# Token numbers copied in FFN units, turn counts loaded once per pair, third row group used from unit 12

## What is computed

```
q_p, k_p = phi(q), phi(k)            # phi: [exp(xW - m), exp(-(xW - m))], m = max|xW|
attn = (q_p @ (k_p.T @ v)) / (q_p . sum(k_p) + 1e-6)
e_idx = argmax(x @ w_gate)           # x = attn; one of 8 experts for each token
out[tokens of e] = gate * sigmoid(x @ w_output_gate)[e] * (relu(x @ w1[e]) @ w2[e])
xn = x / rms(x) * rms_g              # second layer: x = out, d_ff = 1536
y  = (silu(xn @ w_gate) * (xn @ w_val)) @ w_out
```

## Time and profile before

| | us |
|---|---|
| median of 3 runs | 875.22 |
| lowest, highest | 873.22, 879.47 |
| the profiled execution | 873.63 |
| its span | 871.9 |
| attention and routing | 0 to 214 |
| experts' steps | 214 to 445 |
| FFN units | 445 to 730 |
| output tiles | 730 to 872 |

### The profile page before, as it was taken

The page is one execution under the profiler, slowest core; times in us unless marked ns, Lnnn a source line. Parts: engine busy times, 40 slices in busy tenths (PEclk is TensorE's granted clock), DMA queues, the critical chain, the costliest instruction groups (busy, mean ns, idle before and its releaser), DMA issues.

```text
span 871.9 us, 16594 instructions
## 1 busy us (share of the span) xinstructions
PE 840.2 (96%) x6216; PEld 757.3 (87%) x6217; DVE 538.9 (62%) x934; ACT 347.3 (40%) x547; POOL 161.4 (19%) x169
## 2 busy tenths in 40 slices
PE   8999999998988999999989999999999999999997
PEld 6685867767988999999989999999999998888885
DVE  5688786989766954445569777666765774212210
ACT  4544454573155533322354443333433443212211
POOL 1010302112350433203421031111110000101101
PEclk9999999999999999999999999999999999999999
DMA  8613713112349544554662852232421945343320
GB/s 285 209 57 138 275 54 108 55 38 75 127 175 267 227 114 97 141 148 150 184 230 77 280 180 79 79 80 79 142 71 54 357 150 184 123 139 125 125 101 36
DMA packets 65226, 122.41 MB, mean 140 GB/s; under 512 B 9200, under 2 KB 43120, under 8 KB 62480
## 3 DMA queue, kind: packets, MB, share of 16 engines
q1 hardware_dynamic: 57600, 91.98, 34.3%
q0 software_dynamic: 3488, 17.85, 5.3%
q10 hardware_dynamic: 4080, 11.80, 3.9%
HBM read 77.54 MB, written 44.09 MB: 139 GB/s over the span
## 4 chain that ended last, share of the span: by engine, by line
PE 78%; DVE 11%; issue 6%; DMA 2%; ACT 1%; DVEq 1%; SPq 0%; another core or an unknown queue 0%; POOLq 0%; POOL 0%; ACTq 0%
PE ps L1207 9%; PE ps L1209 9%; PE ps L1208 9%; PE ps L1259 5%; PE ps L1258 5%; PE ps L1260 5%; PE ps L956 3%; PE ps L1115 3%; PE ps L1116 3%; PE ps L1117 3%; PE ps L1128 3%; PE ps L1130 3%; PE ps L1129 3%; PE ps L1011 3%; PE ps L916 2%
## 5 line engine op out<-in xcount | busy, mean ns | idle before, releaser
L1207 PE MATMUL ps<-sH,tb 128*128 128x384 f32 x504 | 171.0, 339 | 5.9 <-DVE val L2018 2.9
L1208 PE MATMUL ps<-sL,tb 128*128 128x384 f32 x504 | 170.0, 337 | 0.0
L1209 PE MATMUL ps<-sH,tb 128*128 128x384 f32 x504 | 169.9, 337 | 0.0
L1207 PEld LDWEIGHTS ps<-sH,tb 128*128 128x128 f32 x504 | 95.0, 189 | 8.5 <-DVE val L2018 4.9
L1208 PEld LDWEIGHTS ps<-sL,tb 128*128 128x128 f32 x504 | 95.1, 189 | 0.1
L1209 PEld LDWEIGHTS ps<-sH,tb 128*128 128x128 f32 x504 | 95.2, 189 | 0.0
L2036 DVE TENSOR_TENSOR hTL<-h_st,hTH 128x768 fp32r<-128x768 f32 x36 | 33.0, 954 | 97.4 <-ACT hTH L1516 97.4
L1260 PE MATMUL ps<-woH,hTL 128*128 128x512 f32 x216 | 84.1, 389 | 0.0
L1259 PE MATMUL ps<-woL,hTH 128*128 128x512 f32 x216 | 84.1, 389 | 0.0
L1258 PE MATMUL ps<-woH,hTH 128*128 128x512 f32 x216 | 84.0, 389 | 0.0
L1115 PE MATMUL ps<-xmH,w1H 128*128 128x288 f32 x256 | 76.8, 300 | 5.9 <-issue 2.8
(11 more groups left out here) (246 smaller groups left out, 1784.8 us busy)
## 6 DMA issues: line engine op xcount, KB each, us to landing
h_dram<-hid SPq DMA_DIRECT2D x36, 384.0 KB, 2.8
h_st<-h_dram SPq DMA_DIRECT2D x18, 768.0 KB, 4.1
t_dram<-tb SPq DMA_DIRECT2D x6, 1792.0 KB, 5.7
t_raw<-in_ffn_up SPq DMA_DIRECT2D x13, 512.0 KB, 3.2
tb<-t_dram ACTq DMA_DIRECT2D x6, 1024.0 KB, 6.7
xin<-xs_dram SPq DMA_DIRECT2D x9, 578.2 KB, 9.3
xs_dram<-zrow SPq DMA_DIRECT2D x8, 578.2 KB, 7.9
qT<-in_q SPq DMA_DIRECT2D x4, 1152.0 KB, 5.8
```

The costliest lines, as they stand in the source:

```text
L1207: e.matmul(to, wh, xh, start=(fresh and c == 0), stop=False, skip_group_check=True)
L1208: e.matmul(to, wh, xl, start=False, stop=False, skip_group_check=True)
L1209: done = e.matmul(to, wl, xh, start=False, stop=(c == 1), skip_group_check=True)
```

## The change

1. **Counts.** `turn_of` becomes `turns_of`: both turns' counts are loaded at the begin of a pair (4 loads, on VectorE 5), and none between a pair's turns.
2. **SP's step.** `rows_out(n)` now stands ahead of `step_weights_in(n+2)`, and `numbers_out` is out of the loop.
3. **Numbers.** They are copied at units 6, 8, ... 20, one step each, right behind that unit's `hidden_out`; further steps, if there are any, at unit 21. The numbers are read at unit 23 (before 15) and converted at unit 25 (before 17).
4. **Begin of the FFN.** `group_in(0)` ahead of `operands_in(0)`; `operands_in(1)` waits for the first high part (`s_hi0`) in place of the last hidden chunk.
5. **Around unit 4.** `rows_out(last)`, its waits and `group_in(2)` now stand ahead of `hidden_out(4)`.
6. **Order of units.** (3,0) (3,1) (4,0) (4,1) (5,0) (5,1) (3,2) (4,2) (5,2) in place of (3,0) (3,1) (4,0) (4,1) (3,2) (4,2) (5,0) (5,1) (5,2): group 2 is used from unit 12. Its splits move by two units (from 8A..10B to 10A..12B). `MADE_AT[6]` goes from 13 to 14, and the raw load of visit 6 now follows unit 12 in place of unit 10.
7. **Semaphores.** The sums have one semaphore per group. Group 2's sums stay on GpSimd, with the same waits.

```diff
-MADE_AT = {6: 13, 7: 16, ...
-UNITS = ([(v, sg) for sg in range(2) for v in range(3)] + [(3, 0), (3, 1), (4, 0), (4, 1), (3, 2), (4, 2)]
-         + [(v, sg) for v in range(5, 9) for sg in range(NSG)]
+MADE_AT = {6: 14, 7: 16, ...
+UNITS = ([(v, sg) for sg in range(2) for v in range(3)] + [(v, sg) for v in range(3, 6) for sg in range(2)]
+         + [(v, 2) for v in range(3, 6)] + [(v, sg) for v in range(6, 9) for sg in range(NSG)]
...
+NUMBERS_AT = tuple(range(6, 6 + 2 * (NTOK // G), 2))
...
-        def turn_of(e, x):
-            tiles = e.value_load(tab[0:1, bass.ds(x + TILES, 1)], ...)
-            first = e.value_load(tab[0:1, bass.ds(x + FIRST, 1)], ...)
-            return tiles, first
+        def turns_of(e, pair):
+            return [(e.value_load(tab[0:1, bass.ds(pair * 2 + (par + TILES), 1)], ...),
+                     e.value_load(tab[0:1, bass.ds(pair * 2 + (par + FIRST), 1)], ...))
+                    for par in range(2)]
...
             with e.Fori(0, pairs) as pair:
-                for par in range(2):
-                    tiles, first = turn_of(e, pair * 2 + par)
+                counts = turns_of(e, pair)
+                for par, (tiles, first) in enumerate(counts):
                     with e.If(tiles > 0):
...
                 rows_next(n + 2)
                 weights_out(n + 1)
+                rows_out(n, column_of(n))
                 step_weights_in(n + 2)
-                rows_out(n, col)
-                numbers_out(n, col, row)
...
-            e.wait_ge(s["e_st"], 16 * 8)
-            operands_in(0)
             e.wait_ge(s["xst"], total * 16)
             group_in(0)
-            rows_out(prior, prior_col)
-            e.wait_ge(s["pe_s1"], total * FC)
+            e.wait_ge(s["e_st"], 16 * 8)
+            operands_in(0)
+            rows_out(prior, column_of(prior))
+            e.wait_ge(s["s_hi0"], 1)
             operands_in(1)
...
             for u in range(NU):
-                hidden_out(u)
                 if u == ROOT_AT + 1:
                     rows_out(last, last_col)
                     e.wait_ge(s["s_lo"], 7)
                     e.wait_ge(s["xst"], total * 16 + 32)
                     group_in(2)
+                hidden_out(u)
...
+                if u in NUMBERS_AT:
+                    n = NUMBERS_AT.index(u)
+                    if n > 0:
+                        e.wait_ge(s["idst"], n * 16)
+                    e.dma_start(ids_dram[bass.ds(column_of(n), G), :], xs_dram[bass.ds(row_of(n), G), DM:DM + 1])...
```

More of the change, by code:

```diff
@@ L307, in build_program @@
             "FFN up weights of a step: loaded, sums, operands split, stored": "e_in e_add e_hi e_lo e_st",
-            "FFN rows loaded (one per group), their sums, operands split": "x_in0 x_in1 x_in2 s_add s_add1 s_hi0 s_hi s_lo",
+            "FFN rows loaded (one per group), their sums, operands split": "x_in0 x_in1 x_in2 s_add0 s_add1 s_add2 s_hi0 s_hi s_lo",
             "FFN up operands loaded (two parts per buffer)": "t_a0 t_a1 t_a2 t_b0 t_b1 t_b2",
@@ L413, in piece_of @@
             return w1[:, n, :] if n < KC else w2[:, 2 * (n - KC):2 * (n - KC) + 2, :].rearrange("p c n -> p (c n)")
-        def turn_of(e, x):
-            tiles = e.value_load(tab[0:1, bass.ds(x + TILES, 1)], min_val=0, max_val=NTOK // G)
-            first = e.value_load(tab[0:1, bass.ds(x + FIRST, 1)], min_val=0, max_val=NTOK // G + E)
-            return tiles, first
+        def turns_of(e, pair):
+            return [(e.value_load(tab[0:1, bass.ds(pair * 2 + (par + TILES), 1)], min_val=0, max_val=NTOK // G),
+                     e.value_load(tab[0:1, bass.ds(pair * 2 + (par + FIRST), 1)], min_val=0, max_val=NTOK // G + E))
+                    for par in range(2)]
         def is_early(e):
@@ L460, in sums_done @@
         def sums_done(sg, n):
-            return (s["s_add1"], n) if sg == 1 else (s["s_add"], 4 * (sg // 2) + n)
+            return s[f"s_add{sg}"], n
         def nth_load(v):
@@ L579, in rows_next, with numbers_out @@
                 rows_in(row)
-            def numbers_out(n, col, row):
-                e.wait_ge(s["idst"], n * 16 + 16)
+            def numbers_out(n):
+                e.wait_ge(s["idst"], n * 16)
                 settle(e, "carry_sp")
                 with nc.allow_non_contiguous_dma(reason="token numbers"):
-                    e.dma_start(ids_dram[bass.ds(col, G), :], xs_dram[bass.ds(row, G), DM:DM + 1])\
+                    e.dma_start(ids_dram[bass.ds(column_of(n), G), :], xs_dram[bass.ds(row_of(n), G), DM:DM + 1])\
                         .then_inc(s["idst"], 16)
@@ L669, in _ @@
             operands_in(2)
-            last_col, last_row = column_of(last), row_of(last)
+            last_col = column_of(last)
             for u in range(NU):
-                hidden_out(u)
                 if u == ROOT_AT + 1:
@@ L681, in _ @@
                         weights_in(vis)
[L682 to L687, removed]
+                if u in NUMBERS_AT:
+                    n = NUMBERS_AT.index(u)
+                    if n > 0:
+                        e.wait_ge(s["idst"], n * 16)
+                    with nc.allow_non_contiguous_dma(reason="token numbers"):
+                        e.dma_start(ids_dram[bass.ds(column_of(n), G), :], xs_dram[bass.ds(row_of(n), G), DM:DM + 1])\
+                            .then_inc(s["idst"], 16)
+                if u == NUMBERS_AT[-1] + 1:
+                    with e.If(total > NTOK // G):
+                        with e.Fori(NTOK // G, total) as n:
+                            numbers_out(n)
+                if u == NUMBERS_AT[-1] + 3:
+                    e.wait_ge(s["idst"], total * 16)
                     settle(e, "carry_sp")
@@ L857, in row_sums @@
             def row_sums(sg, half):
[L859 to L860 removed]
+                x, to, done = xst[sg], s_sum[sg], s[f"s_add{sg}"]
                 if half == 0:
                     e.wait_ge(s[f"x_in{sg}"], 16)
[L863 to L865 removed]
+                    e.tensor_tensor(to[5][:, :, :], x[:, 0:2, GN:2 * GN], x[:, 2:4, GN:2 * GN], ALU.add).then_inc(done, 1)
+                    e.wait_ge(done, 1)
+                    e.tensor_tensor(to[3][:, :, :], to[5][:, :, :], x[:, 0:2, 0:GN], ALU.subtract).then_inc(done, 1)
                     return
[L867 to L869 removed]
+                e.wait_ge(done, 2)
+                e.tensor_tensor(to[2][:, :, :], x[:, 2:4, 0:GN], to[3][:, :, :], ALU.subtract).then_inc(done, 1)
+                e.tensor_tensor(to[4][:, :, :], x[:, 0:2, 0:GN], x[:, 0:2, GN:2 * GN], ALU.subtract).then_inc(done, 1)
             total = total_steps(e)
@@ L1964, in turns @@
                 with e.Fori(0, pairs) as pair:
[L1965 to L1968, removed]
+                    counts = turns_of(e, pair)
+                    after_pair = e.value_load(tab[0:1, bass.ds(pair * 2 + (TILES + 2), 1)], min_val=0, max_val=NTOK // G)
+                    for par, (tiles, first) in enumerate(counts):
+                        nxt = counts[1][0] if par == 0 else after_pair
                         with e.If(tiles > 0):
@@ L2039, in beside @@
             def beside(u, pos):
+                for sg, n in SUM_AT.get((u, pos), ()):
+                    row_sum(sg, n)
                 for sg, o in LOW_AT.get((u, pos), ()):
```

45 lines of the change are left out of this document (17 added, 28 removed).

## The result

The changed kernel takes 881.12 us in the median of 20 runs (878.69 to 885.14). The kernel before, run in turns with it, takes 876.86. The ratio is 1.0049, with an interval of 1.0036 to 1.0062: slower by 4.3 us (3.2 to 5.4). The forecast was slower by 3.7, "within 1%".

What follows compares the result with a forecast made beforehand. TensorE, busy 96% of the span, bounds the kernel, so time is its work plus gaps. Gains of 6.9 us and losses of 10.6 net +3.7 on the median 875.22, giving 878.9 us; range 869 to 886.

Steps and rivals of the forecast that it cites:

- Unit 4: Unit 4's store, issued behind group 2's load, lands late and delays TensorE's wait for val in unit 8: loss 6.0 us.
- Rival 1: Unit 4's store isn't late, so the loss of 6.0 becomes 0: 872.9 us; chance 0.17.
- rival 2: DMA queues share the engines, so unit 8's gap is 3.2 in place of 5.8: 876.3 us; chance 0.10.
- FFN's begin: Without VectorE's count loads, the 2.52 us gap before the first FFN unit and its clock fall go: gain 3.8 us.
- Rival 4: Something else holds VectorE at the FFN's begin, so the gap at 447.81 stays: 882.7 us; chance 0.08.
- First and third turn: TensorE's four count loads in place of two lengthen the gaps to 3.0 and 1.9 us: losses 2.2 and 1.4.
- rival 3: More clock falls, at the first and third turn and longer behind unit 8's gap: 883.2 us; chance 0.15.
- SyncE's step: In the steps, storing rows ahead of the next weights' load ends TensorE's 1.83 us wait for x2g: gain 1.8 us.
- seven gaps: TensorE's gaps at three turns, for x2g, at the last step's end, before the FFN and in unit 9: together 9.2 us.
- Unit 1: VectorE's sums in unit 1 wait for group 1's later load and meet GpSimd's squares: loss 0.7 us.
- Visit 6: Visit 6's raw load follows unit 12's last product, so GpSimd sums in unit 14 beside ScalarE's split: loss 0.3 us.
- theory B: Set up for the experiments: the clock's falls are the cost, wherever a gap sets them off; no size or chance given.

Runs made afterwards that it cites:

- e2: The kernel before with only the last rows' store and group 2's load put ahead of unit 4's store; ratio 1.0086 to the kernel before.
- e3: The kernel before with only the counts of both turns loaded at a pair's begin, on all engines; ratio 1.0029 to the kernel before.
- e8: The kernel before with only the rows' store put ahead of the next weights in SP's loop; ratio 0.9964 to the kernel before.
- e1: The changed kernel with unit 4's store put back ahead of group 2's load; ratio 0.9979 to the kernel before.
- e5: The changed kernel with unit 4's store back ahead of the group load and TensorE's counts loaded turn by turn; ratio 0.9916 to the kernel before.
- e7: The changed kernel with unit 4's store first, TensorE's counts loaded turn by turn and group 2's sums on VectorE; ratio 0.9878 to the kernel before.
- e4: The changed kernel with TensorE alone loading its counts at every turn again; ratio 1.0015 to the kernel before.
- e9: The changed kernel with unit 4's store first and the order of units, group 2's splits and MADE_AT[6] as before; ratio 0.9961 to the kernel before.
- e7b: The same kernel as e7, measured once more in another group of runs; ratio 0.9918 to the kernel before.
- e6: The changed kernel with group 2's four sums on VectorE instead of GpSimd, the store still late; ratio 0.9999 to the kernel before.
- e11: The kernel of e7 with the numbers copied in the steps' loop again, as before; ratio 0.9892 to the kernel before.
- e10: The kernel of e7 with operands_in(1) waiting for the last hidden chunk again, as before; ratio 0.9879 to the kernel before.

## Why the prediction was right, step by step

The forecast was +3.7 us, and +4.3 (3.2 to 5.4) was measured. The chain that costs most was foreseen step by step. That the net came within 0.6 us is luck in part: for the three parts measured alone the prediction has +6.0, -0.9 and -1.8, together +3.3, and they came out as e2 +7.5, e3 +2.5, e8 -3.1, together +6.9. The parts not measured alone (the FFN's first loads, the order of units) would have to give the other -2.6, and the errors of the three, some 3.5 us together, cover that. The parts also aren't independent: e3's loss holds 1.9 us more of waiting for `x2g`, a wait that the order of e8 takes away and after doesn't have. What was predicted by rows, and what came:

- **Unit 4, the step weighed most: right in its chain, and the size of its gap too small.** Forecast 6.0; e1 gives 6.1 (3.7 to 8.5) and e2 7.5 (5.0 to 10.0). `xn` was forecast to land at 502.1 and did at 502.7; the load to be issued then, and it was (502.76). But it took 9.8 us, not the 7.0 of the earlier trace rows. The forecast let one store stand behind the load; with the swap there are two, unit 4's and unit 5's, 0.6 and 1.3 us behind it. In the load's time the 16 engines moved 2.81 MB, where in the kernel before they moved 2.16 in 7.0 us (ACT's queue had 15.1% and 14.1% of them): at the 309 GB/s of before, the 0.65 MB more are 2.1 of the 2.8 us. The store then landed 1.1 us behind it, not 2.2, the two products took 5.0 us, not 4.3, and the gap was 8.5, not 5.8. The clock was at half for 10.2 us, not 3.4: at 17 matmuls in 5.55 us, where the full rate of the same profile (28 in 4.40) gives 2.7 us for 17, that is 2.9 lost, not 1.7. The old gap of unit 9 (1.54) didn't return, as forecast. Marks around the unit give 9.5 us for this one execution, which lies 1.8 above its median.
- **Rival 1 (the store isn't late) and rival 2 (the queues share) are out.** From 495 to 499 us SyncE's queue had 2.0% of the engines, ACT's 95.6%, though `xn` had been issued at 493.92. The rule of the Trainium skill weighed in the prediction (DMA: Bandwidth & Descriptors, queues, rings and completion order) isn't seen here either; what holds SyncE's queue back isn't shown.
- **FFN's begin: right.** Forecast 3.8 of 4.2. No gap, full clock at 448 us, and the 0.4 kept for the fifth operand wasn't there in after; e5 and e7 have it (0.36 and 0.35). Rival 4 is out. The chain of waits of after has no load of VectorE between 443 and 447 us.
- **First and third turn: the gaps right, the clock half right.** Forecast 3.0 and 1.9, measured 3.11 and 1.99. The second turn's 0.7 went. The clock fell behind both, with 16 matmuls in 3.3 us, where the kernel before has 27 in 3.4 at the first turn (245.4 to 248.8): 1.3 us lost each time, in place of the 0.85 and nothing that were counted. The third turn's fall was rival 3's. For these gaps the prediction's terms give a gain of 2.2 + 1.4 = 3.6 when TensorE's loads go back, less 0.7 if the second turn's gap returns, which it didn't; e4 measured 3.0 (0.9 to 5.1).
- **SyncE's step: right.** Forecast 1.8, measured 3.1 (1.3 to 4.9) in e8. In after the gap went, but the wait for `hmL` in that step grew from 1.1 to 1.5: something else was late next. The prediction left that wait out of its seven gaps, and another of 1.38 for `xmL` at 216.25; all of TensorE's waits from 214 to 730 us come to some 15 us, not 9.2.
- **Unit 1: right.** Forecast +0.7. Its gaps went from 0.50 and 0.59 to 1.33 and 0.45, as VectorE waits 1.36 us for group 1's load. **Visit 6: right**, a gap of 0.32 in unit 15 for 0.3, though by the marks the units from 9 on take no longer in sum.
- **What did not hold is the use made of "the gaps of 1.83 us and less had none"**, from which the prediction drew that a short gap is safe. In e1 and e9 gaps of 3.1 and 2.0 us at the turns brought no fall; in after 1.99 did, in e1 1.90 did, and in e3 1.77 did. So the clock's terms can be put down only as a chance, and theory B is true in part: falls are in the sum, but behind gaps that had other causes, and where the gaps went (e5, e7) the falls went too. The mean clock over all executions says the same: 0.989 in after, 0.994 to 0.995 in the kernel before, 0.998 to 0.999 in e5, e7 and e7b.
- **The forecast's 878.9 us itself** is 2.2 below the 881.12: it was put on a median of three executions of the kernel before, 875.22, which with 20 became 876.86. Only the difference is comparable.

What stays open: what decides whether a gap of 2 to 3 us brings the clock down, and how long the group load takes. All four kernels with the late store (after, e2, e4, e6) have two stores within 1.3 us behind the load, and it took 9.2 to 9.8 us. Where the second store comes 6.8 us behind or later (before, e3, e5, e7, e7b, e8, e11), it took 7.0 to 7.4. That fits the bytes above. But in e1, e9 and e10 the second store comes 3.8 to 6.4 us behind, and the load took 8.4 to 9.7, which the bytes don't explain. No run took these apart.

## What to carry to other kernels

Two issues swapped on one DMA queue can cost more than all that a change wins: before putting a large load ahead of a small store, find who needs the store's buffer, and price the load with all that will then be queued beside and right behind it: the same 1536 KB took 7.0 to 9.8 us in these runs. Work that a load releases on GpSimd starts when the load lands, so look at what VectorE does just then; moving the sums to free slots of VectorE took away the collision. Register loads cost where nothing else is left to do behind them: putting VectorE's early took away the gap ahead of the FFN, and leaving TensorE's spread over the turns was better by 3.0 us.

## What the hardware did that was not expected

- **VectorE and GpSimd take turns by whole instructions.** Products with both inputs in SBUF took 2.55 and 2.44 us beside GpSimd's sums and 0.96 without, and GpSimd's own sums went from 1.80 to 2.40 and 2.52. In the rows each waits for the other's instruction to end: the product issued at 514.60 ended at 517.15, 0.8 us behind the sum that had begun at 514.54 (to 516.34), and the sum issued at 516.42 ended 1.7 us behind that product. `val`, with one input in PSUM, stayed at 0.96 beside a sum (519.73). The Trainium skill (SBUF — State Buffer, "SBUF: two separate sides") says that the two engines' shared pair of ports is locked for a whole instruction, and for a VectorE operation without a performance mode only if it has two SBUF inputs and GpSimd reads SBUF. The trace agrees as far as it goes; every sum here reads SBUF, so the case of a GpSimd operation that doesn't is not seen.
- **How long the clock stays low goes with the gap.** Behind gaps of 1.8 to 3.7 us it was 3.4 us; behind 5.25 (e6) and 7.47 (e2) 6.8; behind 7.7 (e4) and 8.49 (after) 10.2. Part of that time passes within the gap itself and costs nothing: in after, 4.65 of the 10.2 us.
- **Whether a short gap brings it down differs from one execution to another.** The gap of 2.5 us at the FFN's begin did in the kernel before, and did not in e8, where the window behind it (447.6 to 451.0) shows 1.00.
